# Where the gates are turned and the first expert's second weights are awaited, at the seam between two stages

## The reference

```
# attention-like recurrence over 768 steps -> x [3072, 384]
h = x @ w_in;  x = (h - tanh(h)) @ w_out           # feed-forward, 2048 wide
logits = normalised(x) @ normalised(expert_emb).T / tau
expert_idx = argmax(logits);  gate_w = softmax(logits)[expert_idx]
for e in range(8):                                  # 8 experts, 384 -> 1024 -> 384
    mask = expert_idx == e
    out[mask] = gate_w[mask] * (relu(x[mask] @ w1[e]) @ w2[e])
```

## Time and profile before

| | us |
|---|---|
| median of 3 runs | 842.95 |
| lowest, highest | 841.18, 843.7 |
| the profiled execution | 841.18 |
| its span, first to last instruction | 839.4 |
| PE busy | 818.4 (97% of the span) |
| DVE busy | 642.2 (77%) |
| ACT busy | 506.8 (60%) |
| POOL busy | 218.5 (26%) |
| mean granted TensorE clock | 0.988 of full |

### The profile page before, as it was taken

One profiled execution on the slowest core, in us unless ns is written; L12 is line 12 of the kernel. 1 busy time (PEld: TensorE's weight loads), 2 busy tenths in 40 slices (PEclk: granted clock), 3 DMA queues, 4 the chain that ended last, 5 costly groups with the idle time before them and its releaser, 6 DMA issues. The chain is left out here.

```text
span 839.4 us, 18150 instructions
## 1 busy us (share of the span) xinstructions
PE 818.4 (97%) x5840; PEld 744.5 (89%) x5841; DVE 642.2 (77%) x983; ACT 506.8 (60%) x1057; POOL 218.5 (26%) x239
## 2 busy tenths in 40 slices
PE   8999989999999999999999999898999999999995
PEld 7777768889999999999999998798999999999994
DVE  8999859999998998998998997825545464647552
ACT  5766777767667667666666766224545463646652
POOL 6534424321111111111111332123223222232211
PEclk9999999999999999999999999989999999999998
DMA  9989943225234224223323676289596769693440
GB/s 232 287 273 287 295 125 95 66 76 182 96 109 161 89 99 163 99 88 125 137 93 118 223 243 238 94 305 392 217 332 237 268 228 389 243 351 118 178 162 9
DMA packets 86429, 157.89 MB, mean 188 GB/s; under 512 B 8059, under 2 KB 23565, under 8 KB 86384
## 3 DMA queue, kind: packets, MB, share of 16 engines
q1 hardware_dynamic: 58672, 100.82, 36.5%
q10 hardware_dynamic: 23744, 45.69, 15.2%
q0 software_dynamic: 3968, 10.82, 3.6%
HBM read 117.97 MB, written 40.70 MB: 189 GB/s over the span
## 5 line engine op out<-in xcount | busy, mean ns | idle before, releaser
L1306 POOL TENSOR_TENSOR ew_l<-ew_raw,ew_h 128x512 fp32r<-128x512 f32 x48 | 62.4, 1299 | 272.3 <-DVE poly L1524 268.0
L1226 PE MATMUL y_ps<-wout_h,g_h 128*128 128x392 f32 x384 | 130.8, 341 | 0.4 <-DVE g_l L1515 0.4
L1227 PE MATMUL y_ps<-wout_l,g_h 128*128 128x392 f32 x384 | 130.4, 340 | 0.0
L1228 PE MATMUL y_ps<-wout_h,g_l 128*128 128x392 f32 x384 | 130.4, 340 | 0.0
L1226 PE MATMUL h_ps<-xT_h,win 128*128 (+1 forms) x288 | 113.4, 394 | 1.2 <-DVE diff L1505 0.8
L1228 PE MATMUL h_ps<-xT_h,win 128*128 (+1 forms) x288 | 113.4, 394 | 0.0
L1227 PE MATMUL h_ps<-xT_l,win 128*128 (+1 forms) x288 | 112.8, 392 | 0.0
L1701 DVE SCALAR_TENSOR_TENSOR ex_hT_l<-e_bank,ex_hT_h 128x512 fp32r<-128x512 f32 x48 | 33.2, 691 | 104.0 <-ACT ex_hT_h L1957 104.0
L1524 DVE COPY_PREDICATED poly<-large,diff 128x512 f32<-128x512 uint8 x96 | 72.0, 750 | 17.5 <-DVE poly L1520 17.5
L1858 PE MATMUL e_bank<-ex_xT_h,w_ex 128*128 128x256 f32 x288 | 82.7, 287 | 2.4 <-issue 2.4
L1859 PE MATMUL e_bank<-ex_xT_l,w_ex 128*128 128x256 f32 x288 | 82.3, 286 | 0.0
(11 more groups left out here) (244 smaller groups left out, 1993.5 us busy)
## 6 DMA issues: line engine op xcount, KB each, us to landing
w_raw<-in_w ACTq DMA_DIRECT2D x26, 1536.0 KB, 11.2
ew_raw<-in_w SPq DMA_DIRECT2D x48, 256.0 KB, 2.7
w_h<-ew_h SPq DMA_DIRECT2D x48, 256.0 KB, 2.3
w_l<-ew_l SPq DMA_DIRECT2D x48, 256.0 KB, 2.0
w_ex<-w_h SPq DMA_DIRECT2D x8, 1536.0 KB, 7.5
w_ex<-w_l SPq DMA_DIRECT2D x8, 1536.0 KB, 12.8
kv_sb<-in_kv SPq DMA_DIRECT2D x24, 384.0 KB, 6.3
krT_sb<-in_krT SPq DMA_DIRECT2D x44, 192.0 KB, 6.2
```

Of the source, the lines that this page charges most:

```text
L1226: pe.matmul(out, lh, rh, start=start, stop=False)
L1227: pe.matmul(out, lh, rl, start=False, stop=False)
L1228: return pe.matmul(out, ll, rh, start=False, stop=stop)
L1306: pool.tensor_tensor(ew_l[:, slot, :], raw, ew_h[:, slot, :].bitcast(F32), ALU.subtract).then_inc(ew_l_made, 1)
```

## The change

Five edits, all around the seam between routing and experts:
1. Expert 0's second weights: both halves are issued together in the last block of the last group (`f == KF - 1`), where the high half was issued at block 10 and the low half at block 14.
2. `keep_warm` before the token numbers has 28 products for 24, the one after them 20 for 15.
3. `turn_gates(pe, 0)` moves from the end of routing to behind the barrier, after `transpose_tokens(0)`; `turn_gates(pe, NT // 2)`, which raises `gates_turned`, moves from there to behind `first(0)`.
4. `take_gates` on DVE moves from ahead of step 0 to behind `hidden_low(0)`.
5. On SP `pass_expert(e - 1)` stands behind `load_expert(e)`; expert 0 was passed first of all, ahead of the wait for `gates_turned`.

```diff
@@ route_tensor
-            keep_warm(pe, h_ps[1], ident, 24)
+            keep_warm(pe, h_ps[1], ident, 28)
...
-            keep_warm(pe, h_ps[1], ident, 15)
-            turn_gates(pe, 0)
+            keep_warm(pe, h_ps[1], ident, 20)
@@ feed_forward, SP
-                        if last and f == HALF + 2:
-                            sp.wait_ge(h_done, KF * (CH - 1) + HALF)
+                        if last and f == KF - 1:
+                            sp.wait_ge(h_done, KF * CH)
...
-                            load_second(sp, w, w2_h, w2_l, w_loaded, 0, (0,))
-                        if last and f == KF - 2:
-                            sp.wait_ge(h_done, KF * CH)
-                            load_second(sp, w, w2_h, w2_l, w_loaded, 0, (1,))
+                            load_second(sp, w, w2_h, w2_l, w_loaded, 0)
@@ experts, SP
-                pass_expert(0)
                 sp.wait_ge(gates_turned, 1)
                 for t in range(2):
                     sp.wait_ge(gathered[2 + t], 16)
                 for e in range(1, E):
                     load_expert(e)
-                    pass_expert(e)
+                    pass_expert(e - 1)
+                pass_expert(E - 1)
@@ experts, DVE
                     hidden_low(u)
+                    if is_first(u):
+                        take_gates()
...
-                take_gates()
                 steps(dve, step)
@@ experts, PE
                     first(u, par)
+                    if is_first(u):
+                        turn_gates(pe, NT // 2).then_inc(gates_turned, 1)
...
                 transpose_tokens(0, 0, 0)
-                turn_gates(pe, NT // 2).then_inc(gates_turned, 1)
+                turn_gates(pe, 0)
                 steps(pe, step)
```

More of the change, by code:

```diff
@@ L181, in second_weights, with load_second @@
     return w[:, 2 * WIDE:6 * WIDE].rearrange("p (s h f) -> p s h f", s=2, h=2)
-def load_second(eng, w, w2_h, w2_l, w_loaded, e, halves=(0, 1)):
-    for half in halves:
-        src = (w2_h, w2_l)[half]
+def load_second(eng, w, w2_h, w2_l, w_loaded, e):
+    for half, src in enumerate((w2_h, w2_l)):
         eng.dma_start(second_weights(w)[:, e % 2, half, :].bitcast(F32).rearrange("p (a f) -> p a f", a=NP),
```

## The result

| | before | after |
|---|---|---|
| median | 843.09 | 851.37 |
| lowest, highest of 4 runs each | 841.18, 843.7 | 849.54, 853.24 |
| the profiled execution | 841.18 | 855.25 |
| its span | 839.4 | 853.5 |

After over before is 1.0102, with a 95% interval from 1.0073 to 1.0133: 8.3 us slower. The forecast was 846.0 with a range up to 848.4, so it had the sign and not the size.

A forecast was written before the change was run, and what follows sets the result against it. PE's idle time and clock were taken as the bound. `second(1, 0)` 2.85 us later from expert 1's weights, less 1.4 won up to T, is +1.45; with 1.7 of low clock, +3.1 us: 846.0, range 841.5 to 848.4.

The forecast's parts named there:

- What bounds the kernel: Whole kernel: PE is busy 818.4 of 839.4 us, so only PE's idle time and clock can give or take.
- Up to T, -1.4 us: Routing and `first(0)`, whose end is T (T' after the change): 1.4 us shorter, between -0.1 and -3.4.
- DVE is the floor: Barrier after routing: DVE reaches it at 544.23 and limits the gain, so it comes 0.4 us earlier (0.1 to 0.6).
- The 0.3 us to be won in the gate products: Gate products behind the transposes: at most 0.45 us comes back from the low clock; 0.3 taken.
- The 0.7 us of clock in `first(0)`: `first(0)`: the low clock costs 2.3 us there; between 0 and 2.3 comes back, 0.7 taken.
- Expert 0's weights, 0: Last group's end: issuing both halves one or two blocks later costs nothing; without cover up to 8 us.
- The new wait in step 0, 1.8 us: Ahead of `second(0, 0)`: PE idles 1.8 us until SP raises `w_ready`; bounds 1.5 and about 5.
- No idle time ahead of first(1): Step 0: PE's 2.43 us of idle time go, and with them 1.7 us of low clock in `first(1)`.
- Expert 1's weights at T' + 24.2: Ahead of `second(1, 0)`: weights issued later land at T' + 24.2; PE idles 3.8 us, net +1.45 us.
- The low clock behind it, 1.7 us: After the wait ahead of `second(1, 0)`: PE's clock falls, adding 1.7 us.
- (2): Rival at `second(1, 0)`: expert 1's weights land in time, by T' + 20.5; -1.7 us; chance 0.13.
- (3): Rival on SP: its issues block some 3 us, first wait 5 us, expert 1 lands 3 later; +6 us; chance 0.07.

The follow-up runs named there:

- gates_half_behind: Kernel before with edit 2 and only the first half of the gate products moved behind the barrier, the second half still ahead of `first(0)`; 843.3 us.
- after_e0_early: Kernel after without edit 1: expert 0's second weights issued at blocks 10 and 14 as before; 850.2 us.
- after_warm: Kernel after with 28 products instead of 20 in the second `keep_warm`, nothing else changed; 849.5 us.
- after_pass_first: Kernel after without edit 5: expert 0 is passed first, ahead of the wait for `gates_turned`; 853.3 us from three runs.
- only_gates: Kernel before with only the second half of the gates moved behind `first(0)` and `take_gates` moved (edit 4); 850.5 us.
- half_hold_warm: Kernel before; `keep_warm` 28 and 24, first gate half behind barrier, ACT's solo loads behind unit 1's high part, SP's expert 2 load held until they land; 838.1 us.

## Why the prediction was wrong, point by point

- **What bounds the kernel**: right. All of the loss is PE's idle time and PE's clock.
- **Up to T, -1.4 us**: wrong, +1.3 in the profiled execution; this is the first step that failed. The barrier was to come 0.4 us earlier "and DVE is the floor". The floor is POOL, 2.4 us behind the issue of its second gather, a resource that the sum didn't name; PE's work was taken away there, the barrier came no earlier for it (S + 25.6 in gates_half_behind and 25.5 in after_e0_early, for 25.4), and PE's gap grew from 0.87 to 3.52 us. And edit 1, "Nothing", made the transposes 1.2 us later. The 0.3 us to be won in the gate products went the other way, 0.7 us lost with the transposes, since the clock was low from the transposes on. The 0.7 us of clock in `first(0)` came back as forecast (10.1 us for 10.8); that this is the very number is partly luck, since after_e0_early and after_warm, with the same `first(0)`, had no low clock there at all.
- **Expert 0's weights, 0**: wrong, about 1.2 us. PE's own need of them was covered, as the forecast said. The transfers queued beside them were not looked at.
- **The new wait in step 0, 1.8 us**: it measured 1.28, below the bound of 1.5. SP issued 1.26 us after T', not 2.2. The gate products end at 566.68 and SP issues at 566.72, 0.04 later, where I took 0.7 from the end of unit 0; why that row is longer stays open. By itself this wait costs nothing, since the later one absorbs it (after_pass_first).
- **No idle time ahead of first(1)**: right, and the low clock behind it was gone as well. The clock fell in `second(0)` instead, from 569.1 to 572.4, which the forecast had named as absorbed by the later wait. It was: PE was ready for `second(1, 0)` at T' + 22.1, for a forecast 20.7, and expert 1's weights came 5 us behind that.
- **Expert 1's weights at T' + 24.2**: this is the second step that failed. The mechanism was right and the term too small; they landed at T' + 27.2, and PE waited 5.28 us for a forecast 3.8. They were issued 0.9 us earlier than reckoned. But the sum began the transfer 1.3 to 3 us after issue, and it was nearly 5. The view of the DMA queues of the kernel after shows it, first of 570.5 to 571.5, then of 571.5 to 572.5 (q10 is ACT, q1 SP; packets, MB, share):

```profile
q10 hardware_dynamic: 196, 0.40, 102.9%
```

```profile
q10 hardware_dynamic: 107, 0.22, 56.2%
q1 hardware_dynamic: 93, 0.19, 49.8%
```

  SP's first DMA, issued at 566.72, has no byte moved until 571.5, while ACT's queue has the engines for itself; from 572 on both move the same. The two shares add up to one, as in the earlier trace rows. The Trainium skill, DMA: Bandwidth & Descriptors, section Queues, rings and completion order, has each DMA engine take turns between the rows that have work; from 572 on this agrees with the row, and for the five microseconds before, the row shows that SP's queue did not count among them. The trace of before had this too: expert 2's pair, issued at 568.86, moved nothing until 572.5.

  From its first byte the pair took 21.1 us, where the sum had 19.2. SP's queue had moved 3.57 MB by then, 0.42 more than the pair: part of expert 2's, issued at 578.81, went ahead of the pair's last bytes. That isn't the cause, though: in only_gates, where expert 2 was issued only after the landing, the pair took 22 us from its first byte, and its last 0.26 MB took 4.3 of them. Why the end is so slow stays open.
- **The low clock behind it, 1.7 us**: right, 1.8.
- **The sum**: +3.1 forecast. The landing 2.9 late and T' 2.7 late are 5.6 of the 6.2 us that were missing in the profiled execution (9.3 less 3.1). Another 0.3 is a slip of the sum: it says that 581.02 is the second product of `second(1, 0)` but counts from it, so PE had been ready there at T + 21.4 and not T + 21.65, and the way from `first(1)` to there had taken 10.0 us and not 10.3. In the medians T' is likely nearer to the forecast: after is the slowest of its executions. How the clock fell in the four timed runs no trace tells.
- **The rivals**: (2), in time, asked for a landing by T' + 20.5 and was off by 7 us; the middle of its sum is -1.5 and not -1.7. (3), a blocked issue on SP, had nearly the right total, +6, by a mechanism that didn't occur. No case had the routing get longer, so the range ended at 848.4.

The forecast's range was too narrow because the sign of the routing term was taken as settled; its bounds, -0.1 to -3.4, held no loss at all, though the floor of the barrier had been read off one engine only. The landing, 2.8 us beyond its upper bound of T' + 24.4, was the other half.

## What to carry to other kernels

Before a transfer's issue is moved behind a computation, add up all bytes that are wanted in the same stretch: here 3.1 MB that had been moved while the DMA engines were idle were put beside 4.7 MB of others, and 6 us came of it. Look for the cost of a later DMA at the transfers next to it, not only at its user. Work that fills an engine's wait ahead of a barrier is worth more than the time it takes when the clock falls behind the gap: with four more products that nobody reads the median was 3.3 us lower (half_hold_warm). What ends a barrier must be read on every engine, GpSimd too, and in more than one trace. And a blocked DMA issue swallows what is won ahead of it, so the blocked issue is what has to be moved first.

## What the runs showed of the hardware

- ACT's issue of two DMAs of 1.5 MiB blocks ACT while earlier ones are under way: 3.92 us before, 6.16 in gates_half_behind, 1.70 in after. It ended 10.1 to 10.9 us after SP's issue of expert 1's pair in the nine executions in which SP had issued 4 to 6.4 us ahead, however early ACT's began.
- Of SP's and ACT's queues the one that comes second into the DMA engines waits some microseconds for its first byte, and the first has them for itself: in after SP's issue at 566.72 moved nothing until 571.5; in before ACT's at 560.04 nothing until 563.5, and SP's at 568.86 nothing until 572.5. Issued into idle engines at 554.79, SP's first byte came within 1.2 us, and the pair's second half landed 12.6 us after its own issue. With more beside it that took 17.1, 21.5 and 25.3 to 26.3 us.
- POOL lets the barrier go 2.4 us after its last indirect DMA's issue ended; PE 0.45 us after its last product. The transposes came 2.6 to 2.7 us after POOL's issue in every execution in which PE was not the last, and 0.47 to 1.7 after DVE's last row.
- The same code up to T took between 37.3 and 42.2 us from S in two executions, by where the granted clock fell. One profiled execution is not enough to price a term of a few us there.
